# Two reorderings around a feed-forward stage and an expert stage: first halves of two tiles ahead of their second halves, and a slot's transposes ahead of another slot's scores

## The reference

```
# 1. gated linear attention, over t:  S = a_norm[t] * S + k[t] (x) v[t];  y[t] = q[t] @ S.re
# 2. feed-forward with a convolution over tokens
h = np.maximum(x @ w_in, 0.0)                         # 384 -> 1024
conv_out += conv_w[k][None, None, :] * hp[:, k:k + S, :]      # 3 taps
x = (h * (1.0 / (1.0 + np.exp(-conv_out)))) @ w_out   # 1024 -> 384
# 3. four causal attention "experts" of width 64; each token uses the best two of four
for e in range(E):
    q, k, v = x @ wq[e], x @ wk[e], x @ wv[e]
    a = softmax(where(causal, -1e9, scale * (q @ k.transpose(0, 2, 1))))
    out += gate[e] * (a @ v @ wo[e])
```

## Time and profile before

| | |
|---|---|
| runs before, median (lowest to highest of 3) | 769.32 us (765.98 to 770.83) |
| profiled execution, its own time | 768.88 us |
| its span, first to last instruction | 767.0 us |
| mean granted TensorE clock | 0.991 of full speed |
| busy: TensorE / its weight loads / VectorE / ScalarE | 665.8 / 513.8 / 617.1 / 406.2 us |

### The profile page before, as it was taken

How to read it: one execution, slowest core, us unless ns; L and a number is a source line. 1 busy time by engine, 2 the same in 40 slices (tenths; PEclk the granted TensorE clock), 3 DMA queues, 4 the chain that set the end, 5 groups by cost and what they waited for, 6 DMA issues and landing times.

```text
span 767.0 us, 13207 instructions
## 1 busy us (share of the span) xinstructions
PE 665.8 (87%) x5244; PEld 513.8 (67%) x5244; DVE 617.1 (80%) x1164; ACT 406.2 (53%) x743; POOL 0.2 (0%) x4
## 2 busy tenths in 40 slices
PE   0000995999999999999999999999999999999998
PEld 0000884876656788876656788876667788998765
DVE  3999885899989878899888878899888675763563
ACT  6303246533657855533757755434766434754565
POOL 0000000000000000000000000000000000000000
PEclk9999997899999999999999999999999999999999
DMA  8604890410017563400029563400037440000001
GB/s 345 253 0 121 224 254 23 165 42 0 1 41 199 174 188 85 173 34 1 0 62 247 174 160 103 146 1 0 2 103 206 126 119 9 1 0 1 2 21 43
DMA packets 93565, 73.85 MB, mean 96 GB/s; under 512 B 8640, under 2 KB 85696, under 8 KB 92864
## 3 DMA queue, kind: packets, MB, share of 16 engines
q1 hardware_dynamic: 93504, 73.01, 31.5%
HBM read 49.34 MB, written 23.65 MB: 95 GB/s over the span
## 4 chain that ended last, share of the span: by engine, by line
PE 51%; DVE 37%; ACT 8%; issue 3%; DMA 1%; SPq 0%; DVEq 0%; ACTq 0%
DVE cv L1110 8%; PE wide L1539 5%; PE wide L1390 5%; PE wide L1520 5%; PE bank L1590 5%; PE wide L1574 4%; PE bank L1598 4%; PE wide L1402 4%; DVE m L928 3%; DVE heads L1115 3%; DVE m L927 2%; PE wide L1515 2%; DVE W L940 2%; DVE nmax L1174 2%; PE wide L1511 2%
## 5 line engine op out<-in xcount | busy, mean ns | idle before, releaser
L1455 PE MATMUL wide<-x_hi_lo,win_hi 128*128 128x384 f32 x384 | 108.0, 351 | 1.3 <-DVE x_hi_lo L1074 1.3
L1377 PE MATMUL wide<-ident,heads 96*128 96x96 f32 x160 | 18.7, 265 | 75.8 <-DMA heads<-heads_dram 75.8
L1476 PE MATMUL wide<-heads,wout 128*128 128x384 f32 x200 | 70.7, 496 | 4.9 <-DVE heads L1115 4.9
L1174 DVE TENSOR_REDUCE nmax<-wide 128x1 f32<-128x768 f32 (+2 forms) x96 | 55.2, 616 | 23.6 <-PE wide L1548 23.4
L1455 PEld LDWEIGHTS wide<-x_hi_lo,win_hi 128*128 128x128 f32 x384 | 70.4, 189 | 5.3 <-issue 3.2
L1110 DVE SCALAR_TENSOR_TENSOR cv<-h,wconv,cv 128x768 f32<-128x768 f32 x64 | 64.8, 1012 | 8.2 <-ACT cv L669 6.6
L1377 PEld LDWEIGHTS wide<-ident,heads 96*128 96x128 f32 x160 | 16.6, 154 | 76.2 <-issue 76.2
L1539 PE MATMUL wide<-attn 64*128 64x512 f32 (+3 forms) x256 | 65.0, 482 | 2.3 <-ACT attn L693 2.3
L717 ACT ACTIVATE xs<-wide 128x896 f32<-128x896 f32 x48 | 44.1, 918 | 41.8 <-PE wide L1574 41.8
L1455 PE MATMUL wide<-x_hi_lo,win_lo 128*128 128x384 f32 x192 | 64.9, 338 | 0.0
L674 ACT ACTIVATE cv<-cv 128x768 f32<-128x768 f32 x32 | 27.1, 846 | 59.3 <-DVE cv L1110 59.1
(11 more groups left out here) (193 smaller groups left out, 1479.9 us busy)
## 6 DMA issues: line engine op xcount, KB each, us to landing
heads<-heads_dram SPq DMA_DIRECT2D x96, 192.0 KB, 3.6
araw<-a_in SPq DMA_DIRECT2D x12, 768.0 KB, 5.9
araw<-qk_in SPq DMA_DIRECT2D x12, 768.0 KB, 4.8
heads_dram<-m SPq DMA_DIRECT2D x20, 384.0 KB, 3.6
heads_dram<-araw SPq DMA_DIRECT2D x20, 384.0 KB, 3.5
v<-v_in SPq DMA_DIRECT2D x4, 1536.0 KB, 7.2
out_dram<-h SPq DMA_DIRECT2D x24, 192.0 KB, 2.1
wout<-w_out_t SPq DMA_DIRECT2D x1, 1536.0 KB, 10.7
```

Source lines behind the costliest of these rows:

```text
L1174: dve.tensor_reduce(nmax[:, t, side:side + 1], slot_scores(t, side), AXX, ALU.max, negate=True).then_inc(s_nm, 1)
L1455: last = MM(low[u % 2][:, 0:NT], w[:, k, mt * P:(mt + 1) * P], xs[:, k, n * NT:(n + 1) * NT], start=(k == 0 and part == 0), stop=(k == KT ...
L1476: last = MM(mlp_bank[u][:, 0:NT], wout[:, mt, k * P:(k + 1) * P], hgate(mt)[:, n * NT:(n + 1) * NT], start=(mt == 0), stop=(mt == MT - 1))
```

## The change

It reorders two places and alters no computation. A list `H_ORDER` sets the order of the sixteen half tiles: (0,0), (1,0), (0,1), (1,1), then as before. The banks, the waits and ScalarE's `relu` calls follow that list. In the expert stage slot 0 is transposed before the scores of slot 2 are made; later slots keep their order.

```
+H_ORDER = [(0, 0), (1, 0), (0, 1), (1, 1)] + [(mt, n) for mt in range(2, MT) for n in range(NN)]
...
-            def relu(b, mt):
-                if mt == 1:
+            def relu(b, mt, n):
+                u = H_ORDER.index((mt, n))
+                if mt == 1 and n == 0:
                     act.wait_ge(s_ff, b + 1)
...
-                act.wait_ge(s_hr, NN * (MT * b + mt) + NN)
+                act.wait_ge(s_hr, NN * MT * b + H_ORDER.index((mt, NN - 1)) + 1)
...
-                    relu(b, mt)
+                    for u, (tile, n) in enumerate(H_ORDER):
+                        if tile == mt and mt > 1 or mt < 2 and u < 4 and (u == 3) == mt:
+                            relu(b, tile, n)
...
-                u = NN * mt + n
+                u = H_ORDER.index((mt, n))
...
-                h_products(b, 0, 0)
-                for mt in range(MT):
-                    for n in range(NN):
-                        if (mt, n) != (0, 0):
-                            h_products(b, mt, n)
-                    if mt >= 2:
+                for mt, n in H_ORDER:
+                    h_products(b, mt, n)
+                    if n == NN - 1 and mt >= 2:
                         mlp_products(b, mt - 2)
...
                 for t in range(SLOTS):
+                    if t == 0:
+                        transpose_probs(b, t)
                     if t + 2 < SLOTS:
                         expert_scores(b, t + 2)
-                    transpose_probs(b, t)
+                    if t:
+                        transpose_probs(b, t)
```

More of the change, by code:

```diff
@@ L643, in relu @@
                     act.wait_ge(s_hg, MT * b + mt - 1)
-                for n in range(NN):
-                    u = NN * mt + n
-                    act.wait_ge(s_h, NN * MT * b + u + 1)
-                    nc.scalar.activation(h[:, mt % 2, 1 + n * NT:1 + (n + 1) * NT], low[u % 2][:, 0:NT],
-                                         ACT.Relu).then_inc(s_hr, 1)
+                act.wait_ge(s_h, NN * MT * b + u + 1)
+                nc.scalar.activation(h[:, mt % 2, 1 + n * NT:1 + (n + 1) * NT], low[u % 2][:, 0:NT],
+                                     ACT.Relu).then_inc(s_hr, 1)
             def w_out_hi(i):
```

## The result

| | before | changed |
|---|---|---|
| median (lowest to highest of 4 runs each) | 769.88 us (765.98 to 770.83) | 777.44 us (776.04 to 778.06) |
| ratio, 95% interval | 1 | 1.012 (1.0077 to 1.0163) |
| profiled execution: its own time, span | 768.88, 767.0 us | 776.04, 774.3 us |

The change costs 7.6 us here by the medians and 9.2 by the ratio, between 5.9 and 12.5 by its interval; the forecast was 4.1.

What follows compares the result with a forecast made beforehand. The prediction took VectorE's full list, released through ScalarE's `first_tap`, to bound stage 2 of batches 0 to 2. Adding 3.25 us (half tiles) and 0.85 us (transposes) to 768.88 gave 773.0 us, range 769.0 to 777.5.

Steps and rivals of the forecast that it cites:

- Part 1: Half tiles of tiles 0 and 1: filler outlasts TensorE's pause and delays VectorE's list; 3.25 us slower over four batches.
- Part 2: Experts, slot 0's transposes first: scores of slot 2 reach VectorE later; 0.85 us slower over four batches.
- the two sizes on TensorE named above: Experts: slot 0's transposes put at 0.91 us, TensorE's next turn at 2.12 us after the last projection.
- the difference of 0.24: Experts: scores of slot 2 begin 0.24 us later per batch in batches 0 to 2.
- The clock rival: Batch 3, first second-layer product: TensorE's pause grows to 2.9 us and its clock falls; 775.6 us, chance 0.27.
- which cost it half of that, 2.6 us: Earlier pause of 3.90 us: 5.2 us of TensorE work at half clock cost 2.6 us, the price assumed for batch 3.
- The faster rival: Both changed places: TensorE, the fullest engine, sets the end, so removed pauses gain 4.8 us; 764.1 us, chance 0.06.
- The sum: Whole kernel: 3.25 plus 0.85 makes 4.1 us slower, 773.0 us.
- with the 2 us or so by which the shown runs differ from their median: Whole run: allowance for spread used to set the forecast range, 769.0 to 777.5 us.

Runs made afterwards that it cites:

- small_filler: Kernel before, with only 3 of the 9 matmuls of half tile (1,0) put into TensorE's pause before (0,1): 770.16 us, ratio 1.0001.
- again: The changed kernel, unedited, measured a second time: 773.18 us, ratio 1.0074 of before.
- again2: The changed kernel, unedited, measured a third time: 774.06 us, ratio 1.0066 of before.
- not_last: Kernel before, with the new half-tile order in batches 0 to 2 only, expert stage as before: 773.51 us, ratio 1.0051.
- h_only: Kernel before, with the new half-tile order in all batches, experts in the old order: 776.51 us, ratio 1.0104.
- t_only: Kernel before, with only slot 0's transposes moved ahead of the scores of slot 2: 769.69 us, ratio 1.0011.
- last_only: Kernel before, with the new half-tile order in batch 3 only, expert stage as before: 770.64 us, ratio 0.9989.
- cover_before: Kernel before, with VectorE's idle times filled by norm steps (batches 1, 2) and one product (batches 0 to 2): 764.19 us, ratio 0.9927.
- cover_small: Kernel before, with VectorE's idle times filled and 3 matmuls of (1,0) in TensorE's pause: 763.69 us, ratio 0.9917.

## Why the prediction was wrong

**Part 1 held, step by step.** The pause before (0,1) went; the filler outlasts it; `relu`, `first_tap` and VectorE's list move by the difference. Forecast 0.67, 0.79, 0.84, 0.95 = 3.25 us; the profiles of the change and of before differ by 0.68 (counted at the first product of the second layer), 0.80, 0.85, 0.96 = 3.29. Only batch 0 varies from one execution to the next, from about 0.4 to 0.97, with the moment at which the clock is back.

**Part 2** was sized at 0.85 and measures 3 x 0.12 less 0.10 in batch 3: 0.26. In batches 0 to 2 the failing numbers were the two sizes on TensorE named above, each some 0.05 to 0.08 too large, of which the difference of 0.24 was made. That is a warning on small differences: an error of 0.05 in each term is half of the answer. In batch 3 the sign was wrong, since TensorE's own turn comes last there.

**The clock rival** had the right place and pause. The step "which cost it half of that, 2.6 us" failed: 1.0 us is what it costs, in half of the executions, for the fall lasted 3.4 us instead of 5.2 and TensorE is not alone the bound there. Worth 0.5 us on average.

**The faster rival** failed for part 1, as small_filler shows: TensorE's pauses there were worth nothing. It stopped at the 87% of TensorE's products; TensorE's weight loads stand at 67%, below VectorE's 80%.

**The sum** of what is shown is 3.3 + 0.26 + 0.5 = 4.1 us. That this equals the forecast is in part luck: part 2 came out 0.6 lower, and the clock, which the sum had at nothing, 0.5 higher. The two repetitions give 5.7 us (2.9 to 8.4) and 5.1 us (2.2 to 8.0) by their ratios, 5.65 and 3.25 by their medians, and all 28 executions of the changed kernel in the three comparisons average 774.7 us against 769.5 for 100 of the kernel before: +5.2. That is what the change costs as well as it is known, and 4.1 is within both intervals.

**The mean granted clock** of each execution is on record too, for the 28 of the changed kernel and for 96 of the 100 of the kernel before, and it goes with the time (average us, number of executions):

| mean granted clock | before | changed | difference |
|---|---|---|---|
| 0.992 and more | 766.2 (24) | 769.8 (3) | 3.5 |
| 0.990 to 0.991 | 769.3 (21) | 772.2 (5) | 2.9 |
| 0.988 to 0.989 | 769.5 (7) | 773.7 (6) | 4.2 |
| 0.985 to 0.987 | 770.4 (27) | 774.8 (5) | 4.4 |
| 0.981 to 0.984 | 772.7 (17) | 777.3 (1) | 4.6 |
| 0.980 and less | none | 778.5 (8) | |

A line through both sets with one common slope puts the changed kernel 4.0 us above the other at equal clock (3.0 to 4.9), against 3.55 us read from the stretches; a microsecond of full-speed time lost to the clock goes with 0.7 us of time. The three measurements of the changed kernel agree once this is taken off: 4.3 us for the first four runs, 4.1 for again, 3.7 for again2; not_last stands 2.3 us above the kernel before, near the 2.55 of its stretches (0.91, 0.79, 0.85), and h_only 5.1, from six runs only. The rest of the 5.2 us goes with a lower mean clock of the changed kernel, 0.9863 against 0.9886, which is 1.8 us more of full-speed time lost, 1.3 us by that slope. About half of this is the fall in batch 3, 1.7 us lost in half of the executions. Where the other half arises is not shown, and a line through such pairs does not say which of the two, the lost clock or the longer time, brings about the other.

**The step that failed** is that the forecast adds its 4.1 us to one execution, "768.88 + 4.1 = 773.0", as if the clock outside batch 3's pause stayed that execution's (a term put at nothing, with no reason given), and the one on which the chances stood: "with the 2 us or so by which the shown runs differ from their median". The profiled execution of before had a mean clock of 0.991; the first four runs of the changed kernel had 0.987, 0.980, 0.982 and 0.980. An estimate from the slope above: 6.7 us of full-speed time more lost, 4.8 us, and 768.9 + 4.0 + 4.8 = 777.7, where 777.44 was measured. Three runs gave a picture of 2 us where the unchanged kernel's runs spread over 11, from 763.8 to 775.1. In the profiled execution of the change 1.9 us come from the start, which nothing had changed, and 2.1 from a load that was late. With a forecast of 4.1 us and such a spread, a result above 1%, 7.7 us, was far more likely than 0.06; the median of 777.44 lies just at the upper edge of the range. In both repetitions the ratio is under 1%, with intervals that reach 1.1 and 1.04%.

**What stays open:** whether the longer pauses of the changed kernel lower its mean clock beyond batch 3, or whether its executions happened to lie low (h_only with 0.985 and not_last with 0.986, which have part 1 in batch 0 too, lie low as well; t_only and last_only, which do not, have 0.990 and 0.991), since each kernel has one profile; and why the load of `araw` and the first rows of `heads` land at different times from one execution to the next.

**Versions that beat both kernels:** cover_before, 764.19 us, 0.9927 of before (0.9894 to 0.996), and cover_small, 763.69 us, 0.9917 (0.9887 to 0.9947), not told apart from it.

## What to carry to other kernels

Before filling a pause, compare the filler with the pause and look at who waits behind it: here 1.56 us went into a hole of 0.68, ahead of the work that the engine at the end of the chain was waiting for. Fill the idle times of that engine, even if another one is fuller: 3 matmuls in TensorE's pause gave 0.0%, two steps in VectorE's idle times of the feed-forward stage and one more in the experts gave 0.7%. And before trusting a difference of 1% from a few runs, compare the stretches between milestones of both profiles: a difference ahead of the first changed instruction can hardly be the change's. And compare executions at equal mean granted clock: between the highest and the lowest of it the unchanged kernel's average time moved by 6.5 us.

## What the runs showed of the hardware

A pause of 2.89 us of TensorE was followed by half clock in 3 of 6 profiled executions, with the same instructions around it. The fall came between 0.2 us before the work resumed and 1.5 us after; it lasted 3.4 us and cost 1.0. After 1.86 us or less it was not seen in batch 3. In batch 0 it was seen once, in h_only, 0.1 us after a pause of 1.84 us, and cost nothing there; a pause of 2.46 us in batch 1 of *again* had none.

The mean granted clock of an execution and its time go together: in the kernel before 24 executions at 0.992 or more average 766.2 us and 17 at 0.981 to 0.984 average 772.7.

The same loads landed up to 2.4 us apart in three executions of one program, and the first 130 us differed by up to 9 us between kernels that are alike up to there (129.48 to 138.46), with a mean granted clock of 0.92 and 0.80 from 85 us on.
